# Routing merged into the experts' block, with its tables and logits made during attention and its gates inside the loop

## What is computed

```python
# attention, per head: q, k normed by rms, softmax(q k' / 8) v -> x, 1792 rows of 768
xn = x / (norm(x) + 1e-6); en = emb / (norm(emb) + 1e-6)
logits = xn @ en.T / tau
idx = argmax(logits); probs = softmax(logits); gate = probs[idx]
for e in range(8):
    mask = idx == e
    out[mask] = gate[mask, None] * (relu(x[mask] @ w1[e]) @ w2[e])   # w1: 768x1024, w2: 1024x768
h = out @ w_in; out = max(0.01 * h, h) @ w_out                       # w_in: 768x2048
```

## Time and profile before

| what | us |
|---|---|
| median of 3 runs | 1277.14 (1275.7 to 1277.72) |
| the profiled execution's own time | 1274.3 |
| its span, first to last instruction | 1272.2 |
| attention, to the end of the last `x_tok` | 332.2 |
| from there to the first matmul of `product1(0)` | 30.2 |
| experts, from there to PE's last matmul | about 394 |
| feed-forward with the blocks' change | about 516 |

### The profile page before, as it was taken

How to read it: one execution, slowest core, us unless ns; L and a number is a source line. 1 busy time by engine, 2 the same in 40 slices (tenths; PEclk the granted TensorE clock), 3 DMA queues, 4 the chain that set the end, 5 groups by cost and what they waited for, 6 DMA issues and landing times. The chain is left out here.

```text
span 1272.2 us, 21192 instructions
## 1 busy us (share of the span) xinstructions
PE 1204.5 (95%) x6986; PEld 1062.7 (84%) x6986; DVE 876.8 (69%) x1209; ACT 737.1 (58%) x1386; POOL 542.1 (43%) x581
## 2 busy tenths in 40 slices
PE   4999999999559999999999977999999999999998
PEld 3888888888448899889988966999999999999997
DVE  4999999999649999999999964455322145542222
ACT  5999999999657787778777835222321122221111
POOL 7888888886237776776677630000000000000000
PEclk9999999999779999999999997999999999999999
DMA  2344343321014554555453114211322312211132
GB/s 70 87 109 120 100 110 98 85 73 41 15 40 153 209 196 178 187 208 188 172 185 127 38 62 112 62 50 51 97 77 77 91 56 72 67 43 56 50 89 74
DMA packets 99979, 126.45 MB, mean 99 GB/s; under 512 B 28568, under 2 KB 81048, under 8 KB 99872
## 3 DMA queue, kind: packets, MB, share of 16 engines
q1 hardware_dynamic: 92416, 103.07, 26.5%
q0 software_dynamic: 3360, 16.52, 3.7%
q10 hardware_dynamic: 4096, 5.51, 1.3%
HBM read 193.88 MB, written 19.27 MB: 168 GB/s over the span
## 5 line engine op out<-in xcount | busy, mean ns | idle before, releaser
L1015 ACT CAST w_hi<-w_raw 128x768 fp32r<-128x768 f32 (+1 forms) x294 | 249.5, 931 | 13.9 <-DMA w_raw<-moe_w_in 12.7
L1085 DVE TENSOR_TENSOR w_lo<-w_raw,w_hi 128x1024 fp32r<-128x1024 f32 x84 | 186.0, 2249 | 12.1 <-POOL w_lo L904 7.0
L1495 DVE TENSOR_TENSOR out_lo<-out_raw,out_hi 128x384 fp32r<-128x384 f32 x64 | 35.7, 558 | 169.8 <-ACT out_hi L1404 169.8
L904 POOL TENSOR_TENSOR w_lo<-w_raw,w_hi 128x1024 fp32r<-128x1024 f32 x42 | 106.3, 2530 | 93.0 <-ACT w_hi L1015 93.0
L1286 PE MATMUL ps_acc<-yT_hi,in_hi 128*128 128x448 f32 x384 | 142.2, 370 | 2.1 <-DVE yT_lo L1481 2.1
L1316 PE MATMUL ps_acc<-gT_hi,out_hi 128*128 128x448 f32 x384 | 142.6, 371 | 0.0
L1288 PE MATMUL ps_acc<-yT_lo,in_hi 128*128 128x448 f32 x384 | 141.2, 368 | 0.0
L1287 PE MATMUL ps_acc<-yT_hi,in_lo 128*128 128x448 f32 x384 | 141.1, 368 | 0.0
L1318 PE MATMUL ps_acc<-gT_lo,out_hi 128*128 128x448 f32 x384 | 140.4, 366 | 0.0
L1317 PE MATMUL ps_acc<-gT_hi,out_lo 128*128 128x448 f32 x384 | 140.3, 365 | 0.0
L1398 ACT ACTIVATE small_h<-ps_acc 128x448 f32<-128x448 f32 x64 | 34.9, 545 | 181.3 <-PE ps_acc L1288 181.3
(11 more groups left out here) (184 smaller groups left out, 2867.9 us busy)
## 6 DMA issues: line engine op xcount, KB each, us to landing
w_raw<-moe_w_in SPq DMA_DIRECT2D x84, 1536.0 KB
in_raw<-moe_w_in_in SPq DMA_DIRECT2D x32, 384.0 KB, 3.3
out_raw<-moe_w_out_in SPq DMA_DIRECT2D x64, 192.0 KB, 2.4
qk_raw<-q_in SPq DMA_DIRECT2D x48, 112.0 KB, 2.1
qk_raw<-k_in SPq DMA_DIRECT2D x48, 112.0 KB, 2.2
v_raw<-v_in SPq DMA_DIRECT2D x48, 112.0 KB, 2.0
x_rows<-x_tok SPq DMA_DIRECT2D x48, 112.0 KB, 2.5
out_rows<-o_sb ACTq DMA_DIRECT2D x26, 168.0 KB, 2.4
```

Of the source, the lines that this page charges most:

```text
L1015: act.copy(out[:, c, :], raw[:, c, :]).then_inc(s_hi, 1)
L1085: dve.tensor_tensor(w1_lo[:, c, :], w1_raw[:, c, :], w1_hi[:, c, :].bitcast(F32), ALU.subtract).then_inc(s_w1lo, 1)
```

## The change

- The block `routing` is gone; its steps stand at the head of `experts`. One barrier falls away, and item 0's conditional weight loads with it.
- In attention, DVE adds up the logits of each batch of 12 heads once these are done (`batch_logits`, 4 times), and POOL makes the index tables in steps 4 to 8 (`tables`; some are built in the memory of `w2_raw` first, and SP's first weight load waits for that).
- The counts over the token tiles come from products with tables (`tiles_before`, `ones`, `same`) in place of the scan. The 16 products of L631 have 22 columns in place of 66.
- DVE's steps write their intermediate results to PSUM where one of two inputs would else be in SBUF too.
- While DVE routes, ACT splits all of w1 and w2 of item 0 (14 casts), and POOL takes chunks 0 to 3 of w1's low parts, ahead of the gathers. After routing, DVE does `lo1(0)` for chunks 4 and 5 and `lo2(0)` for chunks 0, 2 and 3, and then `x_lo(0)`.
- The rows of a slot are read from `slot_in` and `slot_rows` directly, without the small copies `slot_in` and `slot_out` per item.
- The norms of x: SP loads x back from `x_rows` in 16 tiles (344 KB each) during the loop, ACT squares one in each of bodies 3 to 18, POOL's root and DVE's gate exponents stand in body 19, and the exponential and the gates at the end of the loop.
- DVE's low parts don't wait for POOL's; SP waits for both counts.

```diff
+            def batch_logits(n, u):
+                if n % H != H - 1:
+                    return
+                b = n // H
+                dve.wait_ge(s_xc, n + 1)
+                dve.tensor_reduce(rt["logits"]... [:, :, b, :], x_tok[:, :, b * H:(b + 1) * H, D:X]..., AX.X, ALU.add).then_inc(s_lg, 1)
...
+    def pool1(i):
+        return (0, 1, 2, 3) if i == 0 else (1, 4)
...
+            lo1(0)
             gather(0, 0)
             gather(1, 1)
+            lo2(0)
             def body(n, u):
                 if n >= 2:
+                    lo2(n - 1)
                     store_y(n - 2, u)
                 if n + 2 < items:
                     gather(n + 2, u)
                 if n + 1 < items:
+                    lo1(n + 1)
+                if n == items - 2:
+                    pool.wait_ge(s_xss, J)
+                    pool.tensor_tensor(x_norm[:, :], x_ss[:, :], consts["half"][0:R, 0:J], ALU.pow).then_inc(s_xnorm, 1)
...
+            choice()
+            block_starts()
+            places()
+            rows_of_slots()
+            experts_of_items()
             for c in range(C1):
+                lo1(0, c)
+            for c in range(C2 // 2):
+                lo2(0, c)
+            x_lo(0)
+            for c in range(C2 // 2, C2):
+                lo2(0, c)
...
+                if n == items - 2:
+                    gate_exponents()
             for n in range(items):
                 body(n, n % 2)
+            gates()
             copy_y(items - 2, items % 2)
...
+            def load_x(j):
+                if j > 1:
+                    sp.wait_ge(s_xss, j - 1)
+                sp.dma_start(x_chk[j % 2], x_tiles[:, j, :]).then_inc(s_chk[j % 2], 16)
```

More of the change, by code:

```diff
@@ L29, in attention @@
     V_LAG = 5
+    J = T * B
+    items = rt["free_plus"].shape[1]
+    cols = rt["item_column"].shape[1]
     x_dest = x_rows.rearrange("(p t b) d -> p t (b d)", t=T, b=B)
@@ L820, in experts @@
         y_sb = [sb(f"y_sb{u}", [P, DM]) for u in range(2)]
+        slot_in = sb("slot_in", [P, items], I32)
+        slot_rows = sb("slot_rows", [P, items], I32)
+        hot = sb("hot", [R, J, E], F32R)
+        counts = sb("counts", [P, R], F32R)
+        top = sb("top", [R, J])
+        over = sb("over", [R, E, J])
+        blocks = sb("blocks", [1, E])
+        passed = sb("passed", [R, E, E])
+        start = sb("start", [R, E])
+        ends = sb("ends", [1, E])
+        in_which = sb("in_which", [R, J])
+        beyond = sb("beyond", [R, J, items - 1])
+        in_item = sb("in_item", [R, J, cols], F32R)
+        free = sb("free", [P, items])
+        done_before = sb("done_before", [1, items, E])
+        item_e = sb("item_e", [1, items])
+        item_expert = sb("item_expert", [1, items], I32)
+        item_new = sb("item_new", [1, items], I32)
+        x_ss = sb("x_ss", [R, J])
+        x_norm = sb("x_norm", [R, J])
+        x_inv = sb("x_inv", [R, J])
+        shifted = sb("shifted", [R, J, E])
+        exps = sb("exps", [R, J, E])
+        denom = sb("denom", [R, J])
         ps_x = ctx.enter_context(nc.psum_tensor("ps_xm", [P, 2, 512], F32))
@@ L931, in _, with rank, place @@
         def _(pe):
+            def rank():
+                pe.wait_ge(s_hot, 1)
+                all_hot = hot[:, :, :].rearrange("p j e -> p (j e)")
+                pe.matmul(ps_counts, all_hot, rt["ones"][:, :], start=True, stop=True).then_inc(s_cnt, 1)
+                pe.matmul(ps_rank, rt["before"][:, :], all_hot, start=True, stop=False)
+                pe.wait_ge(s_counts, 1)
+                pe.matmul(ps_tot, counts[:, :], rt["same"][:, :], start=True, stop=True).then_inc(s_tot, 1)
+                pe.matmul(ps_rank, counts[:, :], rt["tiles_before"][:, :, :].rearrange("p j e -> p (j e)"), start=False, stop=True).then_inc(s_rank, 1)
+            def place():
+                for j in range(J):
+                    if j % T == 0:
+                        pe.wait_ge(s_place, j // T + 2)
+                    last = pe.matmul(ps_slot, in_lane[j], in_item[:, j, :], start=j == 0, stop=j == J - 1)
+                last.then_inc(s_put, 1)
             def transpose_x(n, u):
```

659 lines of the change are left out of this document (284 added, 375 removed).

## The result

The kernel after takes **1267.95 us** (median of 4 executions, 1266.97 to 1268.64), the kernel before 1277.43 in the same comparison; the ratio is 0.9928 with a 95% interval of 0.9911 to 0.9945. The profiled execution of after took 1267.65 us (span 1265.9) against 1274.3 (span 1272.2) before.

The account below looks back on a forecast made before the run. PE, busy 330.0 of 330.0 us, bounds the experts' loop; the routing chain bounds the stretch before it. Terms +0.2 - 5.0 - 0.3 + 0 + 3.6 = -1.5 us, so 1277.1 - 1.5 = 1275.6 us, range 1270.5 to 1280.

Parts of the forecast that it names:

- Attention: Stretch to the last x_tok: batch sums on DVE and table steps on POOL cost +0.2 us (0 to +1.7).
- Routing: Head of experts: DVE's chain of steps takes 12.2 us, slot_in ends at 345.6, a gain of 8.1 up to there.
- But POOL, which has issued both gathers by 349.0, turns to two low parts of w2 then.: Head of experts: POOL's parts alternate with DVE's five low parts, delaying x_lo(0) to 357.3 and PE to 357.4; stretch -5.0.
- Whenever POOL starts, both its parts fit in before DVE's last ones: Head of experts: firm sum of 347.8, 2 x 1.84 for POOL, 4.9 for DVE and 0.9 for x_lo.
- Rival (a): DVE-POOL turns cost less: product1(0) at 354.1 (-8.3), end +2.1, sum -6.3, 1270.8; chance 0.18, milder form 0.18.
- The first items: From product1(0) to relu(2): clock +0.2, body 1's work for item 0 gone -0.45, w1's low part -0.1; together -0.3.
- PE's work per item is unchanged and has no gap to close: 0.: Loop of the experts: no change in time, relu to relu 18.35 us throughout.
- The squares and the later loads: Loop: ACT's square of about 1.0 us and w1 loads some 2 us later stay hidden; 0.
- rival d: Squares or later loads open gaps in the loop, adding 5 us, 1280.6; chance 0.05.
- The end of the loop: POOL's root and low parts delay gate_exponents to 737.8, copy_y(18), copy_y(19) and the start of product2(20): +3.6 us.
- the other case: End of the loop: if POOL doesn't hold DVE up, the exponents end at 734.7 and the cost is +2.1.
- The difference that was carried over: Whole kernel: the runs' median lies 2.8 us above the profiled execution of 1274.3, giving a base of 1277.1.

Follow-up runs that it names:

- e12: Kernel after with DVE's six low parts of w2 for item 0 moved from the head of the block back into body 1; 1269.85 us, ratio 0.994.
- e3: Kernel after with POOL's two low parts of w2 for item 0 ahead of the gather of item 1; 1272.0 us, ratio 0.997.
- e7: Kernel after with an unused buffer of 128 bytes between w2_lo and x_g; 1274.3 us in one execution.
- e13: Kernel after with all head work for item 0's w2 (ACT's eight casts, POOL's two low parts, DVE's six) back in body 1; 1272.6 us, ratio 0.997.
- e4: Kernel after with POOL's root behind its last low parts, and gate exponents, exponential and gates behind last casts, copy_y(19) and low parts; 1263.0 us, ratio 0.9905.

## Why the prediction was wrong

**Attention** (+0.2): nothing speaks against it. The last `x_tok` starts at 331.85, before at 331.69, and DVE's first step comes 0.3 later; but this point lies anywhere in 1.6 us from one execution to another, so the agreement on 0.2 is luck.

**Routing** (`slot_in` at 345.6): right, 345.5. The steps that write PSUM took 0.29 to 0.30 us over 128 elements, and `over` (L971), from PSUM to SBUF, 0.29, like their kin in SBUF; no surcharge, so the 65 ns more that the prediction quoted from the Trainium skill (VectorE: DVE Perf Modes, The TRN2 errata) don't show here. The 16 products took 3.6, as they had.

**"But POOL, which has issued both gathers by 349.0, turns to two low parts of w2 then."** This step failed, and with it the 3.4 us of the queue on DVE. The second gather was not out by 349.0: it took 5.13 us, until 353.1, while DVE ran its five low parts without a pause, and it ended 0.84 us behind the last of them. That DVE's run held it `e12` shows: there the run is two low parts long, and the same gather took 2.52 us and ended 0.85 behind it. The rows of before had only gathers of 1 to 1.5 us, and I took that for their price anywhere. "Whenever POOL starts, both its parts fit in before DVE's last ones" was the sentence to doubt: it rests on taking turns, as in the loop, where the other engine already waits when one ends. Rival (a) gave this place as 354.1, from x ready at 353.1; it came at 353.95. `e3` shows that the rest of the working was sound: with POOL's low parts where I had them, 357.98.

**The first items** (-0.3): -0.7; right in sign. All of it lies between relu(1) and relu(2), 18.81 to 18.09: they took the loop's period, as said, but that was 18.10 and not 18.35. Up to relu(1) it took 25.6 in both traces.

**"PE's work per item is unchanged and has no gap to close: 0."** This is the second step that failed, 4.7 us. It reads a busy share of 100% as a bound that only less work can move. The work didn't change, its pace did, since removing four buffers of 32 bytes moved x and h by 128 bytes against the weights. The section on the change has no word of places. `e7` takes all of it away with 128 bytes of nothing. And the gain needs the second half, the lead from splitting w2 of item 0 early (`e13`), which the prediction had counted as hidden work that moves nothing.

**The squares and the later loads** (0, rival d): right. No gap appears on PE in the loop.

**The end of the loop** (+3.6): the mechanism and place were right, the size wasn't: +6.8. In the sum's own terms, counted from relu(20): DVE's nine low parts started 4.3 later (1.8 behind relu(20), before 2.5 ahead of it), where the sum had 3.8. With `h_lo(20)` they took 11.8, where it had 11.0; 0.7 of that was a wait for ACT's high part, which had waited for PE, and PE had begun `product2(19)` only after its wait of 2.9 us and ran at half clock from 726.0 to 729.4. The gates took 1.2 in place of 0.8, since one step of them was held (0.74 us, in `e4` 0.17). So `product2(20)` came 5.3 later and not 3.6. The other 1.5 lies inside `product2(20)`, 9.8 us in place of 8.3: behind another wait of 2.1 us the clock was at half again from 739.7 to 743.1. The sum ends where `product2(20)` starts and has no term for the clock. The recorded price of the other case was wrong, too: with the exponents done at 734.7 in place of 737.8, the same count gives about +0.5 and not +2.1.

**The difference that was carried over.** The prediction took 2.8 us between the median and the profiled execution from the kernel before and added them for the kernel after, where they were 0.3. With every term of the table as measured (-6.3), the sum would still have said 1270.8, just inside the range. Of the 7.65 us between 1275.6 and 1267.95, 4.8 are the terms above, 2.5 are this one, and 0.3 is what the profiled executions differ by outside their traced spans. It comes from resting on one profiled execution, and a quick one.

**Together**: the forecast had the gain of the start too small by 3.6, the loop's missing (4.7, and 0.4 in the first items), and the loss at the end too small by 3.2. Rival (a), 1270.8, was nearest, with the right time for the first product and the wrong reason: DVE wasn't held less by turns, POOL was held in its stead. That its sum, -6.3, is that of the table to the digit is luck: it had 0 for the loop and +2.1 for the end, against -4.7 and +6.8. Of the three outcomes, a clear gain had the second largest chance, 0.38; the size and half of the mechanism behind it were not foreseen.

## What to carry to other kernels

A 100% busy PE still has a pace: read starts of equal products against each other, and when an edit adds or drops a buffer, compare where the operands of the products lie, before and after, before explaining a change in the loop. When forecasting a median from one profiled execution, ask how far that execution lies from its own median. Where two engines can hold each other, what counts is which of them is in a run when the other comes, so price a queue's every instruction at both its free and its held time. Steps that nobody needs soon (here the gates) belong where all three engines wait for PE, not ahead of what PE waits for; that was worth 4.9 us, half as much as the whole change.

## What the runs showed of the hardware that was not expected

- The spacing of matmuls depends on where their operands lie: 0.2267 us for 512 columns with 104448 and 104704 bytes from `w1_hi` to `xT_hi`, 0.2325 to 0.2333 with 104512 and 104576, in fifteen traces. Whether the distance or the place of x and h by itself decides is open.
- Feed-forward, with fixed buffers, moves between two rhythms within one execution, 199 or 195 products per 40 us; it changes at pauses. In after it stayed in the slower one for 60 us more than in before, which is 1.2 us, about the +0.8 of the table. What picks the rhythm is open.
- An indirect transfer on POOL that meets an unbroken run of DVE's low parts can be held to the run's end: 5.13 us (after), 5.88 (`e3`), 6.16 (the store at 726.19). With a shorter run, in `e12`, it ended as much behind the run:

```profile
347.26 2.34 DVE L1058 TENSOR_TENSOR w_lo<-w_raw,w_hi 128x1024 fp32r<-128x1024 f32 x2
...
347.93 2.52 POOL L728 DMA_INDIRECT x_g<-x_rows,slot_in  x1 [0.31 <-issue]
```

  0.84 to 0.92 us lie between the last low part's end and the transfer's in all four. But 40 others of the 42 in after took 1.0 to 1.8 us, many of them in the middle of such runs. Most of these stand 0.2 us behind a low part of POOL's, or right behind such a transfer; the two held ones don't. A store at 739.94, behind 1.9 us without work and inside a run, took 0.99 all the same, so what tells them apart is open.
